# Decayed linear attention and two feed-forward layers: blocks of 512 tokens instead of 384, and an attention that makes its output in the layers' layout

## What is computed

```python
B, H, S, D = 4, 8, 768, 48
state = zeros((B, H, D, D))
for t in range(S):
    state = alpha[:, :, t, :, None] * state + einsum('bhd,bhe->bhde', k[:, :, t], v[:, :, t])
    y[:, :, t] = einsum('bhd,bhde->bhe', q[:, :, t], state)
x = y.transpose(0, 2, 1, 3).reshape(B * S, H * D)      # 3072 tokens x 384
h = x @ w_in;  x = (h * tanh(softplus(h))) @ w_out     # layer 1: 384 -> 2048 -> 384
h = x @ w_in2; x = (h * cos(h)) @ w_out2               # layer 2, same sizes
```

## Time and profile before

| | |
|---|---|
| Median of 3 runs | 964.56 us (962.99 to 966.94) |
| The profiled execution | 963.9 us, of which the span from first to last instruction is 962.2 us |
| Mean granted TensorE clock | 0.994 of full |
| Busy: PE, PEld | 942.1 us (98%), 930.6 us (97%) |
| Busy: DVE, ACT, POOL | 491.3 us (51%), 463.2 us (48%), 423.1 us (44%) |
| DMA | 46.65 MB, mean 48 GB/s |

### The profile page before, as it was taken

One profiled execution on the slowest core, in us unless ns is written; L12 is line 12 of the kernel. 1 busy time (PEld: TensorE's weight loads), 2 busy tenths in 40 slices (PEclk: granted clock), 3 DMA queues, 4 the chain that ended last, 5 costly groups with the idle time before them and its releaser, 6 DMA issues.

```text
span 962.2 us, 15959 instructions
## 1 busy us (share of the span) xinstructions
PE 942.1 (98%) x5924; PEld 930.6 (97%) x5924; DVE 491.3 (51%) x839; ACT 463.2 (48%) x943; POOL 423.1 (44%) x515
## 2 busy tenths in 40 slices
PE   8789999999999999999999999999999999999998
PEld 7689999999999999999999989999999999999997
DVE  7983341534324424424301287666666666667663
ACT  2523333332323323233335586666666666666664
POOL 6884453553545535544525643333333333333332
PEclk9989999999999999999999999999999999999999
DMA  8631121120311211114002410000000000000000
GB/s 221 190 82 34 33 58 42 51 63 13 83 34 34 59 33 52 41 41 124 1 1 75 155 59 26 26 26 26 25 26 26 26 26 25 26 6 21 1 26 25
DMA packets 15213, 46.65 MB, mean 48 GB/s; under 512 B 2144, under 2 KB 5600, under 8 KB 15136
## 3 DMA queue, kind: packets, MB, share of 16 engines
q1 hardware_dynamic: 15136, 45.62, 16.9%
HBM read 36.18 MB, written 9.44 MB: 47 GB/s over the span
## 4 chain that ended last, share of the span: by engine, by line
PE 93%; DVE 2%; issue 1%; DMA 1%; ACT 1%; POOL 1%; POOLq 0%; ACTq 0%; SPq 0%; DVEq 0%
PE bank L367 41%; PE bank L352 41%; PE bank L414 4%; PE bank L393 2%; PE bank L410 2%; PE bank L420 2%; DVE w_lo L652 1%; DMA aqk<-aqk_in 1%; PE bank L430 1%; PE bank L386 1%; DVE decay L604 1%; ACT w_hi L466 0%; DVE probs L624 0%; POOL g_lo L766 0%; DVE inv L611 0%
## 5 line engine op out<-in xcount | busy, mean ns | idle before, releaser
L766 POOL TENSOR_TENSOR g_lo<-g,g_hi 128x384 fp32r<-128x384 f32 x256 | 265.0, 1035 | 439.5 <-ACT g_hi L508 439.1
L367 PE MATMUL bank<-g_hi,w_hi 128*128 128x384 f32 x768 | 260.9, 340 | 2.4 <-POOL g_lo L766 2.4
L367 PE MATMUL bank<-g_lo,w_hi 128*128 128x384 f32 x768 | 257.3, 335 | 0.0
L367 PE MATMUL bank<-g_hi,w_lo 128*128 128x384 f32 x768 | 257.0, 335 | 0.0
L508 ACT ACTIVATE g_hi<-g 128x384 fp32r<-128x384 f32 x256 | 134.5, 525 | 143.0 <-PE bank L367 142.1
L352 PE MATMUL bank<-x_lo,w_hi 128*128 128x384 f32 x768 | 175.3, 336 | 3.6 <-DVE x_lo L645 3.6
L352 PE MATMUL bank<-x_hi,w_hi 128*128 128x384 f32 x768 | 177.8, 339 | 0.0
L352 PE MATMUL bank<-x_hi,w_lo 128*128 128x384 f32 x768 | 175.4, 336 | 0.0
L367 PEld LDWEIGHTS bank<-g_hi,w_hi 128*128 128x128 f32 x768 | 144.4, 188 | 3.6 <-ACT g_hi L508 2.1
L367 PEld LDWEIGHTS bank<-g_hi,w_lo 128*128 128x128 f32 x768 | 144.4, 188 | 0.0
L367 PEld LDWEIGHTS bank<-g_lo,w_hi 128*128 128x128 f32 x768 | 144.2, 188 | 0.0
(11 more groups left out here) (51 smaller groups left out, 811.7 us busy)
## 6 DMA issues: line engine op xcount, KB each, us to landing
aqk<-aqk_in SPq DMA_DIRECT2D x44, 288.0 KB, 4.9
w_raw<-w_in SPq DMA_DIRECT2D x25, 384.0 KB, 3.1
v_sb<-v_in SPq DMA_DIRECT2D x24, 192.0 KB, 2.8
mid<-x_out SPq DMA_DIRECT2D x8, 576.0 KB, 2.8
x_raw<-mid SPq DMA_DIRECT2D x8, 576.0 KB, 3.7
out<-x_out SPq DMA_DIRECT2D x7, 576.0 KB, 2.8
x_out<-w_in SPq DMA_DIRECT2D x7, 384.0 KB, 5.0
aqk<-aqk_in SPq DMA_DIRECT2D x4, 192.0 KB, 4.3
```

The costliest lines, as they stand in the source:

```text
L367: mm = nc.tensor.matmul(acc[m][:, 0:NT], wp[:, f, cols], gp[:, tile % 2, :], start=(f == 0 and n == 0), stop=(f == FT - 1 and n == 2))
L766: nc.gpsimd.tensor_tensor(g_lo[:, tile % 2, :], g[:, tile % 4, :], g_hi[:, tile % 2, :].bitcast(F32), ALU.subtract).then_inc(glo_ready, 1)
```

## The change

- **Blocks.** A block is now 512 tokens: one chunk of 128 of each of the four batches. There are 6 blocks, 96 tiles a layer, 192 in all, and each layer matmul has 512 columns. The attention goes over chunks with the batch innermost, so four states are held (`state[:, b]`).
- **y in x's layout.** `values` makes y directly as features by tokens. The weights are now 32 columns of the state (L333) or of v (L340, L345), and the queries (L333) or `probs` (L340, L345) are streamed, 128 columns each; each product writes a strip of 32 partitions of one bank. It takes 12 products with the state and 16 with `probs` instead of 4 and 8; a head's 48 features are 32 and 16, so the 16 of two heads share a strip, with v padded with zeros (`VH` = 64) and the rows of `w_in` of layer 1 reordered to match. `turn_y`, its copy and its three transposes are gone. The state's update is 8 products of 48 columns by 48 instead of 4 of 112 by 96 (L353), written only where a head's own block lies.
- **Decay by two scans.** A chunk's alphas lie in one row of 516 with a gap in front of each pair. One backward scan makes the products behind each token (`suffix`, L551), a reciprocal of four values a row the starts of the second, forward scan (`growth`, L558). Keys are multiplied by `suffix`, queries by `growth`, one GpSimd instruction of 512 columns each, in place (L698, L704). The carried state is decayed ahead of its use (L711), and the cut to own heads is gone.
- **Order.** `LAG` is 3, one chunk is worked on every four steps, four chunks stand ahead of step 0 with 4 weight pieces, and one piece is split per step after it. The accumulators are copied out by ScalarE (banks 2 and 4) and VectorE (bank 3).

The core of the diff:

```diff
-NT = 384
+NT = BATCH * P
-BLOCKS = TOKENS // NT
+BLOCKS = SEQ // P
-LAG = 4
+LAG = 3
...
+def chunk_at(s, offset):
+    n = s + FT - offset
+    if s >= 0 and n % PER_CHUNK == 0 and n // PER_CHUNK < CHUNKS and s >= offset:
+        return n // PER_CHUNK
+    return None
...
             def values(c):
...
+                if c >= BATCH:
+                    pe.wait_ge(decayed, c - BATCH + 1)
+                    for k in range(KT):
+                        for n in range(4):
+                            p = 2 * k + n // 2 if k < 2 else n
+                            cols = slice(64 * (n % 2), 64 * (n % 2) + 32) if k < 2 else slice(32, 64)
+                            nc.tensor.matmul(turn[32 * n:32 * n + 32, k * P:(k + 1) * P], state[0:ROWS, b, p, cols],
+                                             q_of(c)[0:ROWS, p, :], start=(k == 0), stop=False,
+                                             skip_group_check=True)
+                for k in range(2):
+                    for n in range(4):
+                        h = 4 * k + n
+                        at = 32 * (h % 2)
+                        nc.tensor.matmul(turn[32 * n:32 * n + 32, k * P:(k + 1) * P],
+                                         v_sb[:, c % 3, h, at:at + 32], probs[:, h % 2, h // 2, :],
+                                         start=(c < BATCH and k == 0), stop=True, skip_group_check=True)
+                for i in range(2):
+                    for n in range(4):
+                        mm = nc.tensor.matmul(turn[32 * n:32 * n + 32, 2 * P:3 * P],
+                                              v_sb[:, c % 3, 2 * n + i, 32 - 32 * i:64 - 32 * i],
+                                              probs[:, i, n, :], start=False, stop=True, skip_group_check=True)
...
+                    for p in range(PAIRS):
+                        for i in range(2):
+                            mm = nc.tensor.matmul(to[64 * i:64 * i + D, p * D:(p + 1) * D],
+                                                  kd_t[:, p, 64 * i:64 * i + D],
+                                                  v_sb[:, c % 3, 2 * p + i, 16 * i:16 * i + D],
+                                                  start=True, stop=True)
...
-            def turn_y(c, b):
-                xturn = attn_banks(c)[1]
-                pe.wait_ge(y_ready, at(c + 1, CPS, b))
-                for k in range(KT):
-                    mm = nc.tensor.transpose(xturn[:, k * P:(k + 1) * P], y_sb[:, k * P:(k + 1) * P],
-                                             ident[:, :])
...
+            def grow(c):
...
+                nc.vector.tensor_tensor_scan(after[:, 0:AW][:, ::-1], a_of(c)[0:ROWS, ::-1], first_one[0:ROWS, ::-1],
+                                             1.0, ALU.mult, ALU.add).then_inc(suffix_ready, 1)
...
+                nc.vector.reciprocal(first_inv[0:ROWS, :].rearrange("p (a t) -> p a t", a=PAIRS)[:, :, 0:1],
+                                     after[:, 0:AW].rearrange("p (a t) -> p a t", a=PAIRS)[:, :, 1:2]
...
+                nc.vector.tensor_tensor_scan(growth[0:ROWS, c % 2, :], a_of(c)[0:ROWS, :], first_inv[0:ROWS, :],
+                                             1.0, ALU.mult, ALU.add).then_inc(growth_ready, 1)
...
+            pe.wait_ge(const_ready, 3)
+            warm(14)
+            scores(0)
+            warm(3)
+            scores(1)
+            warm(2)
+            values(0)
+            warm(2)
+            scores(2)
+            values(1)
+            warm(2)
+            scores(3)
+            values(2)
+            warm(4)
+            values(3)
+            warm(4)
```

More of the change, by code:

```diff
@@ L142, in program @@
[L142 to L155, removed]
@@ L456, in _, with step @@
-            run(pe, step)
+            def step(s):
+                if alive(s):
+                    first_product(s)
+                c = chunk_at(s, 2)
+                if c is not None:
+                    values(c)
+                if alive(s - LAG):
+                    second_product(s - LAG)
+                c = chunk_at(s, 0)
+                if c is not None:
+                    scores(c)
+            pe.wait_ge(const_ready, 3)
+            warm(14)
+            scores(0)
+            warm(3)
@@ L459, in _ @@
+            scores(1)
[10 more added lines that the diff above has]
+            warm(4)
+            for s in range(STEPS):
+                step(s)
         @block.scalar
@@ L742, in _ @@
+            dve.wait_ge(scan_const, 4)
+            dve.wait_ge(const_ready, 3)
+            grow(0)
+            grow(1)
+            mask(0)
+            grow(2)
+            mask(1)
+            keep_x_lo(0)
+            grow(3)
+            mask(2)
+            keep_x_lo(1)
+            mask(3)
+            keep_x_lo(2)
             split_w(1)
-            mask(2, 0)
-            keep_x_lo(1, 0)
+            keep_x_lo(3)
+            for c in range(BATCH):
+                add_state(c)
+            grow(4)
@@ L745, in _ @@
             split_w(3)
-            prepare(*prep_chunk(-2), 0)
-            split_w(5)
-            add_state(2, 0)
-            split_w(7)
-            keep_x_lo(2, 0)
-            prepare(*prep_chunk(-1), 0)
-            run(dve, step)
+            for s in range(STEPS):
+                step(s)
         @block.gpsimd
@@ new lines, in prepare, with step @@
+            def prepare(c):
+                keys(c)
+                queries(c)
+                if c >= BATCH:
+                    decay_state(c)
+            def step(s):
+                if alive(s - 1):
+                    g_rest(s - 1)
+                piece = split_at(s)
+                if piece is not None and piece % 2 == 0:
+                    split_w(piece)
+                c = chunk_at(s, 1)
+                if c is not None and c + 1 < CHUNKS:
+                    prepare(c + 1)
```

915 lines of the change are left out of this document (420 added, 495 removed).

## The result

The changed kernel takes 970.73 us (median of 4 runs, 970.70 to 971.55) against 964.61 us (4 runs, 962.99 to 966.94): a ratio of 1.0064, 95% interval 1.0042 to 1.0085. It is slower by a little over half a per cent, a small difference but clear of the scatter between runs, where 918 us had been forecast. The profiled execution took 970.7 us, its span 969.0.

What follows compares the result with a forecast made beforehand. TensorE's instruction stream plus its start was taken as the bound: 30 + 783.4 + 85.4 + 13 + 4.1 = 915.9, plus 1.7 outside the span, gave 917.6, or 918 us, 4.8% below the median; range 880 to 946.

Steps and rivals of the forecast that it cites:

- first layer product: Start of TensorE's layer matmuls, after four chunks are prepared: taken at 30 us, with 26 and 37 as ends.
- layer products: Both layers on TensorE: 3456 matmuls of 512 columns at 226.7 ns, 783.4 us in all, 15.3 us less.
- 20 chunks: Attention on TensorE in the loop: 4.47 us a chunk instead of 5.53, 85.4 us in all against 108.6.
- lost in layer 1: Forecast only as part of 13 us (8 to 20) for losses in the first steps, from late weights and missing stock.
- behind the last product, outside the span: Kernel's end: 4.1 us behind TensorE's last product and 1.7 us outside the profiled span.
- the chain between the products: Layer 2's elementwise passes between first and second products: at most 7.5 us, covered by 12.2 us of other products.
- TensorE busy all the time from 60 us on, with no wait for g_lo, kd or qd: Sign expected in the changed kernel's profile, in both layers, if the forecast was right.
- both rivals on it: 512-column matmul: addition nearly goes, 216.7 ns, 883 us, chance 0.25; or grows with columns, 231.1 ns, 933 us, chance 0.15.
- the 215.8 ns: Trainium skill's value for a 512-column matmul, columns / 2.4 + 2.5 ns; not the one taken.
- The strips work four at a time: y's 56 matmuls in `values`: four column strips side by side, 1.8 us taken, ends 1.54 and 6.2 us.
- the two rivals on strips: y's matmuls: two strips at a time, 944 us, chance 0.12; or none side by side, 1006 us, slower, chance 0.08.
- The decay is off the path in the loop: Two scans of 516, about 2.7 us, run three steps ahead of the scores; costed at nothing.

Runs made afterwards that it cites:

- the first experiment: Changed kernel with one added wait: in layer 2 GpSimd makes g_lo only after the next tile's last angle pass; 911.31 us.
- the seventh experiment: Changed kernel with the angle's last pass reading h from PSUM instead of the middle pass's result from SBUF; 912.39 us.
- the third: Changed kernel with layer 2's gate of tile s-2 instead of s-1, and g_hi of s-2 ahead of ScalarE's turns of s; 959.53 us.
- the fourth experiment: Kernel before (384 columns, LAG 4) with the gate of s-1 instead of s-2 and ScalarE's begin behind the last tile's finish; 1008.23 us.

## Why the prediction was wrong

The sum of the prediction against the profiled execution of the changed kernel. Layer products are 2.04 us each, 192 of the first and 192 of the second kind. Layer 1, up to the first product of layer 2, holds 189 of them (385.6 us), the rest 195 (397.8 us).

| term | forecast, us | measured, us |
|---|---|---|
| first layer product | 30 | 34.1 |
| layer products | 783.4 | 783.4 |
| 20 chunks | 85.4 | 78.5 |
| lost in layer 1 | 13 (both layers) | 507.92 - 34.12 - 385.6 - 78.5 = 9.7 |
| lost in layer 2 | | 964.4 - 507.92 - 397.8 = 58.7 |
| behind the last product, outside the span | 4.1 + 1.7 | 4.6 + 1.7 |
| sum | 917.6 | 970.7 |

**The step that failed** is the one on the chain between the products: "at most 8 x 0.76 + 1.38 = 7.5 us" against 12.2 us of other products, "It is covered". It had three faults.
- It treated the chain as a delay: long enough ago begun, it is covered. That is right for how late a tile may be, and says nothing about how often one can come out. (As a delay it was covered: the first and seventh experiments keep `LAG` 3 and the order, and run at 4.08 us a tile.) What limits the pace is a ring in the order of two engines' programs. Its own numbers would have shown it: gate, three passes of the angle, absolute value and sine are six passes, and six at 0.76 us are 4.6 us a tile, more than TensorE's 4.08. Measured with nothing in the way it is 3.84 us: a slack of 0.24 us a tile, not the 4.7 that 12.2 - 7.5 seemed to leave.
- The part of the diff that closed the ring (gate of s-1 where there had been s-2, on VectorE) has no place in the prediction, which reckons with `LAG` alone.
- It took durations of layer 2 for the wider passes from rows in which GpSimd was seldom beside them: in the kernel before only 16 of the 128 instructions of L685 met a `g_lo`. The earlier trace rows showed what it does to VectorE (5.92 us for 0.90), and the prediction used that for the start alone.

The statement "TensorE busy all the time from 60 us on, with no wait for g_lo, kd or qd" held to 508 us and failed after it. Of TensorE's waits there the profile puts 21.0 us to ScalarE's x_out, the last in a queue that is late, 9.3 us to g_lo, 5.1 of them in the last three, and 4.1 us to VectorE's x_out.

**What held.** The price of a 512-column matmul was right, 226.7 ns, so both rivals on it (216.7 and 231.1 ns) fell, and so did the 215.8 ns that the prediction quotes beside them. The strips work four at a time: y took 1.67 us for 1.8, and the two rivals on strips fell. Together with the update and the changes of mode, `values` costs 2.37 us for 2.80; scores 1.69 for 1.67. The decay is off the path in the loop: its two scans are 1.22 and mostly 2.18 us instead of 2.7 for both, and nobody on TensorE waits for them there. With the ring's stall gone (the first experiment) the kernel takes 911.3 us: the forecast of 917.6, less 6.9 for cheaper chunks, and about 0.6 more elsewhere. That the rest comes out so near is partly luck: its first layer product is 2.6 us later than forecast, and its losses, 8.8 us in layer 1 and 1.8 in layer 2, are 2.4 less. Of the sum's terms only the losses were far off, 68.4 us for 13, and they turned its sign.

**The start** was 4.1 us later than taken, and the stop of 6.16 us behind it was of the kind that the prediction named (VectorE beside GpSimd, weight splits ahead of the attention's work); the losses in layer 1 were within its 8 to 20.

No rival of the prediction was this one. Its slower case was the strips, and that the elementwise engines could set the pace of layer 2 had been ruled out by busy shares, though these were 67% and 66% in layer 2 for VectorE and ScalarE, for tiles of 384 columns.

## What to carry to other kernels

When a change moves an instruction in an engine's order, draw the loops that go through two engines' programs and back, and add up one round of each: the round, not the length of the chain or the busy share, is to be compared with the time of a tile. A ring that is 6% shorter than the pace of the bound engine is one slow instruction away from setting it. And when an order is shifted, ask which instructions now run at the same time: a passing overlap on GpSimd is free until it meets, within such a ring, a VectorE pass that it holds up; here these were passes with two operands in SBUF, and L611 with one.

## What the runs showed of the hardware

**VectorE and GpSimd wait for each other, whole instructions long.** In the changed kernel GpSimd's L691 runs from 643.16 to 644.44 us, and L615, begun at 643.50, ends at 644.99, 0.55 us behind it; that distance is 0.55 us in 95 of the 96 tiles, whether L615 begins 0.34 or 0.62 us into GpSimd's pass. In the other tile its neighbour is a weight split of GpSimd's (L683, 511.57 to 513.40 us), L615 takes 1.98 us, and it ends 0.55 us behind that too. So it isn't slowed in proportion: its end hangs on GpSimd's end, as if it stood still until then. The 5.92 us of the earlier trace rows read the same: GpSimd had three splits one right behind the other, from 28.61 to 33.97 us, and VectorE's, begun at 28.87, ended at 34.79. It did not get in between them. It goes the other way too: here VectorE began first, and GpSimd's L704, 1.18 us elsewhere (25.84), takes 1.81. DVE and POOL of the changed kernel, before layer 1 has got going:

```profile
38.41 2.16 DVE L558 TENSOR_TENSOR_SCAN growth<-shared,first_inv 112x516 f32<-112x516 f32 x1
40.49 0.93 DVE L592 TENSOR_TENSOR w_lo<-w_raw,w_hi 128x768 fp32r<-128x768 f32 x1
...
25.84 1.18 POOL L704 TENSOR_TENSOR g<-g,growth 112x512 f32<-112x512 f32 x1 [1.17 <-DVE growth L558]
...
38.31 1.18 POOL L698 TENSOR_TENSOR shared<-shared,suffix 112x512 f32<-112x512 f32 x1 [2.30 <-DVE suffix L551]
40.65 1.81 POOL L704 TENSOR_TENSOR shared<-shared,growth 112x512 f32<-112x512 f32 x1 [1.17 <-DVE growth L558]
```

The first to start keeps its time and the second waits: the scan L558 loses 0.93 us to L698 that began 0.10 us earlier, and L704 loses 0.63 us to L592. Passes with one operand in PSUM lose nothing (L613, and L615 in the seventh experiment). L611, with a single operand in SBUF, did lose 0.72 us in the third.

The Trainium skill (SBUF — State Buffer, section Who interferes with whom) states this: VectorE and GpSimd have one pair of SBUF ports in common, held by whoever starts first for the whole instruction, and VectorE needs it when it has two SBUF inputs (against a GpSimd instruction that reads SBUF) or runs in a two-port mode, which `tensor_scalar` can. The cases shown here agree with that rule, L611 included, which takes 0.42 us where passes of the same width take 0.69.

**Strips.** Four column strips of 32 work side by side in float32, 30 ns a matmul of 128 columns in place of 110, if the order goes round them; grouped by strip it is 2.39 us for 56 instead of 1.67.

**The clock.** In the changed kernel TensorE fell from 2.4 to 1.2 GHz in the records at or just behind each stop of 4 to 6 us, and came back 7 to 10 us later. So a stop costs more than its length: behind the 4.04 us at a block's end the nine second products took 2.6 us longer, 0.3 of them another wait. Waits of 0.5 to 0.8 us left the clock where it was (the blocks of layer 2 in the third experiment). In between it went both ways: of seven stops of 2.2 to 2.3 us in layer 2 of the fourth experiment four brought the clock down and three did not.
